# Issuing 18 on-chip moves from the sync engine, behind the fourth in-loop weight block, in a fused attention and mixture-of-experts kernel

## What is computed

```
for t in range(768):                     # decayed linear attention, 2 x 8 heads of 48
    y[t] = r[t] @ (state + (u * k[t]) v[t]^T)
    state = w * state + k[t] v[t]^T
x = y as 1536 tokens x 384 features
h = x @ w_in                             # 384 x 2048
x = (max(h, 0) + alpha * min(h, 0)) @ w_out
logits = x @ w_gate                      # 8 experts, the best one for each token, capacity 384
out[token] = gate * (relu(x @ w1[e]) @ w2[e])   # 384 x 1024 x 384 in each expert
```

## Time and profile before

| what | value |
|---|---|
| median of three runs | 447.54 us (447.43, 447.54, 448.78) |
| the profiled execution | 448.75 us |
| its span (first to last instruction) | 446.8 us |
| PE busy | 422.0 us, 94% |
| DVE, ACT, POOL busy | 257.8, 197.1, 176.3 us |
| mean granted TensorE clock | 0.984 of full speed |

### The profile page before, as it was taken

How to read it: one execution, slowest core, us unless ns; L and a number is a source line. 1 busy time by engine, 2 the same in 40 slices (tenths; PEclk the granted TensorE clock), 3 DMA queues, 4 the chain that set the end, 5 groups by cost and what they waited for, 6 DMA issues and landing times.

```text
span 446.8 us, 9384 instructions
## 1 busy us (share of the span) xinstructions
PE 422.0 (94%) x3333; PEld 408.4 (91%) x3333; DVE 257.8 (58%) x555; ACT 197.1 (44%) x450; POOL 176.3 (39%) x189
## 2 busy tenths in 40 slices
PE   5799999999999999999999986899999999998893
PEld 4688889999999999999999985699999999998893
DVE  6898867674445433633437663444568584648820
ACT  2789933432311122111323332344568684558731
POOL 4999625554324432244535861520110311011112
PEclk9999999999999999999999998899999999999998
DMA  7995035437950000000012440494686866564000
GB/s 249 404 353 185 3 112 162 135 94 266 371 199 19 35 1 0 0 35 18 0 35 84 140 148 17 160 352 135 193 229 195 259 197 198 159 213 109 10 19 7
DMA packets 33935, 61.45 MB, mean 138 GB/s; under 512 B 4654, under 2 KB 26910, under 8 KB 33888
## 3 DMA queue, kind: packets, MB, share of 16 engines
q1 hardware_dynamic: 31008, 55.53, 38.6%
q0 software_dynamic: 2880, 5.29, 3.5%
HBM read 47.53 MB, written 14.79 MB: 139 GB/s over the span
## 4 chain that ended last, share of the span: by engine, by line
PE 79%; DVE 7%; ACT 5%; issue 4%; POOL 2%; DMA 0%; POOLq 0%; ACTq 0%; DVEq 0%
PE bank L1154 20%; PE bank L1169 20%; PE bank L1279 18%; PE bank L1308 13%; ACT scores L613 3%; PE bank L1055 2%; PE bank L1266 1%; PE bank L1121 1%; ACT w_high L596 1%; DVE scores L828 1%; DVE neg L886 1%; PE bank L1085 1%; DVE act_full L892 1%; POOL k_hat L484 1%; PE bank L1113 1%
## 5 line engine op out<-in xcount | busy, mean ns | idle before, releaser
L512 POOL TENSOR_TENSOR g_low<-act_full,g_high 128x384 fp32r<-128x384 f32 x63 | 63.6, 1010 | 114.6 <-ACT g_high L642 114.6
L642 ACT ACTIVATE g_high<-act_full 128x384 fp32r<-128x384 f32 x64 | 33.7, 526 | 150.0 <-DVE act_full L892 137.3
L1154 PE MATMUL bank<-x_split,w_high 128*128 (+1 forms) x384 | 98.4, 337 | 0.0
L886 DVE TENSOR_SCALAR neg<-bank,alpha_sb 128x384 f32<-128x384 f32 x64 | 39.2, 613 | 71.5 <-PE bank L1154 71.4
L568 POOL DMA_INDIRECT out<-y_out,token x24 | 25.1, 1047 | 123.8 <-ACT y_out L729 120.1
L1154 PEld LDWEIGHTS bank<-x_split,w_high 128*128 128x128 f32 x384 | 69.0, 188 | 0.2 <-issue 0.2
L1169 PE MATMUL bank<-w_high,g_high 128*128 128x384 f32 x189 | 65.1, 344 | 1.1 <-POOL g_low L512 1.1
L1154 PE MATMUL bank<-x_split,w_low 128*128 (+1 forms) x192 | 64.4, 336 | 0.0
L1169 PE MATMUL bank<-w_high,g_low 128*128 128x384 f32 x189 | 63.8, 337 | 0.0
L1169 PE MATMUL bank<-w_low,g_high 128*128 128x384 f32 x189 | 63.7, 337 | 0.0
L1279 PE MATMUL bank<-xe_high,w_high 128*128 128x256 f32 (+1 forms) x192 | 58.6, 305 | 1.9 <-DVE xe_low L1005 1.9
(11 more groups left out here) (127 smaller groups left out, 793.7 us busy)
## 6 DMA issues: line engine op xcount, KB each, us to landing
w_raw<-chunks SPq DMA_DIRECT2D x96, 192.0 KB, 3.1
w_raw<-chunks SPq DMA_DIRECT2D x32, 384.0 KB, 3.1
rk_in<-att_rk SPq DMA_DIRECT2D x12, 704.0 KB, 6.3
routed_rows<-fill SPq DMA_DIRECT2D x1, 5211.0 KB, 17.1
xe<-routed_rows SPq DMA_DIRECT2D x7, 579.0 KB
v_in<-att_v SPq DMA_DIRECT2D x12, 200.0 KB, 6.2
out<-fill SPq DMA_DIRECT2D x1, 2304.0 KB, 23.4
x_split<-x_split POOLq DMA_DIRECT2D x18, 48.0 KB, 2.6
```

The source lines that it names most:

```text
L512: pool.tensor_tensor(gl[:, f % 4, :], act_full[:, f % 2, :], gh[:, f % 4, :].bitcast(f32), ALU.subtract).then_inc(s_gl, 1)
L642: act.activation(gh[:, f % 4, :], act_full[:, f % 2, :], ACT.Copy).then_inc(s_gh, 1)
L886: dve.tensor_scalar(neg[:, f % 2, :], h, 0.0, alpha_sb[:, f:f + 1], ALU.min, ALU.mult)\
L1154: last = mm(bank[f % 4][:, 0:G], a[:, f, w], x[:, kc, bass.ds(g * G, G)], start=kc == 0 and i == 0, stop=kc == KC - 1 and i == 2)
```

## The change

SP issues the 18 moves in one run, after weight blocks 4 to 7 and ahead of block 8. SP's first loop round is written out (its blocks are constants now), and the loop begins at block 8. POOL issues none of them, and its wait for `s_xl` goes with them. `move_piece`, the order of the 18 and their semaphore stay.

```diff
@@ sync engine
-            with sp.Fori(1, NF // RAW) as k:
+            for m in range(RAW):
+                load_chunk(RAW + m, m)
+
+            sp.wait_ge(s_xl, T)
+            for n in range((NG - 1) * 2 * KC):
+                move_piece(sp, 1 + n // (2 * KC), n % (2 * KC))
+            with sp.Fori(2, NF // RAW) as k:
                 for m in range(RAW):
                     load_chunk(RAW * k + m, m)
@@ gpsimd
             for f in range(NF):
                 g_low(0, f)
-                if f == 0:
-
-                    pool.wait_ge(s_xl, T)
-                for n in range(3 * f // 2, min(3 * (f + 1) // 2, (NG - 1) * 2 * KC)):
-                    move_piece(pool, 1 + n // (2 * KC), n % (2 * KC))
```

## The result

The changed kernel takes 455.34 us in the median of 4 runs (454.74 to 455.78), the kernel before 448.16 in runs beside it (447.43 to 448.79): ratio 1.0162, 95% interval 1.0143 to 1.0181, 7.2 us slower. Forecast were 454.5 (452.0 to 457.2) and +7.0. Its profiled execution has a span of 453.1 against 446.8, 6.3 longer. The four runs of the kernel before fall into two pairs, at 447.4 to 447.5 and at 448.8, and 448.16 is the middle between them. In the 19 to 25 runs of it beside each batch of experiments its median is 447.6 to 447.7; against that the change costs 7.6 to 7.7.

The account below looks back on a forecast made before the run. PE, busy 94% of the span, was taken to bound the kernel. Stall 5.6 plus clock 1.6 minus 0.2 given back made +7.0 us on the median 447.54, so 454.5, range 452.0 to 457.2.

Parts of the forecast that it names:

- What bounds the kernel, and the chain: First group: PE bounds; late block 8 delays ACT, DVE and POOL in turn, then the `down` of step 5, one stall.
- The run of issues: SP between blocks 7 and 8: 18 moves at 0.64 take 11.5 us; block 8 goes out at 78.1, 8.8 late.
- The landing: Block 8 lands 3.1 us after its issue (3.0 to 4.3), at 81.2; ACT wants it at 75.46.
- The stall: PE ahead of the `down` of step 5: it starts at 85.6 instead of 79.96, a stall of 5.6 us.
- The clock: PE's clock halves once after the stall, costing 1.6 us; bounds 0 and 2.8.
- rival (a): Block 8 late, but PE's clock stays up: +5.4 us, 452.9; chance 0.15.
- What is given back: First group after the stall: PE goes at 3.15 against the side loop's 3.19 a step, for -0.2 us.
- POOL's relief: POOL loses 18 issues, 9.5 us in all; worth 0 on the path, at most 0.4 to 0.5 us.
- (b): SP's issues as dear as its first move, 1.02 each with gap: 18.4 us in all, time 461.4; chance 0.08.
- (c): SP's issues cheap, 0.37 a move: block 8 only 0.9 late, 448.3, no measurable change; chance 0.07.
- (d): Block 8 in time, needing 0.32 a move; POOL's relief gains 0.4 to 0.5 us, 447.0; chance 0.04.
- The fills: Two table fills on SP go out at about 97.8 behind block 15 instead of 102.61; cost 0.

Follow-up runs that it names:

- e6: The changed kernel, but with SP's loop written out and block 9 issued only when block 8 has landed: 454.79 us, ratio 1.0152 to the kernel before.
- e8: The changed kernel, but with all 18 moves in one run on SP behind block 15 instead of block 7: 446.89 us, ratio 0.9981 to before.
- e3: The changed kernel, but with 12 moves behind block 7 and the other 6 behind block 15: 449.53 us, ratio 1.0029 to before.
- e2: The changed kernel, but with the same bytes at the same place in 6 wide transfers instead of 18: 450.08 us, ratio 1.0039 to before.
- e5: The kernel before, moves still on POOL, with 18 tiny loads added on SP between blocks 7 and 8: 451.36 us, ratio 1.0082.
- e4: The changed kernel with 44 extra transposes on PE in the stall ahead of the `down` of step 5: 457.29 us, ratio 1.0243 to before.
- e7: The kernel before without the 18 moves anywhere, so groups 1 to 3 have incomplete features: 446.17 us, ratio 0.9973.
- e9: The changed kernel, but with 9 moves on POOL and the other 9 in a run behind block 7 on SP: 447.96 us, ratio 1.0005 to before.
- e10: The changed kernel, but with one move on POOL and 17 spread over SP behind blocks 7 to 15: 446.4 us, ratio 0.9963 to before.
- e1: The changed kernel, but with the 18 moves on SP spread, two behind each of blocks 7 to 15: 446.8 us, ratio 0.9982 to before.

## Why the prediction came out right

**What bounds the kernel, and the chain.** Right, step by step: block 8, ACT's `w_high`, DVE's `w_low`, `neg` and `act_full`, `g_high`, `g_low`, the `down` of step 5. It was one stall, and no later block was late.

**The run of issues.** Forecast 18 x 0.64 = 11.5, SP free at 78.0; measured 11.80, free at 78.26. A single issue took 0.59; one gap of 0.4 in the middle of the run makes most of the difference. The way into the loop was taken for 0.1, for which no row stood, and took 0.50; written out (e6) it is 0.1. Block 8 went out at 78.76 against 78.1.

**The landing.** The term that was mis-sized most: 3.1 forecast, 4.05 measured, inside the bound of 4.3, but that bound came from other rows. It isn't the later blocks (e6). The excess sits in the issue of block 8, 1.18 instead of 0.33; it was long in all three kernels with 18 real moves ahead (0.96 to 1.42), and not with 12, 9 or 18 tiny loads. Block 5's issue and a move inside e8's run were as long, so the count ahead doesn't explain it alone. What SP waits for inside such an issue the trace doesn't name; that stays open.

**The stall.** ACT started on block 8 at 82.83 against 81.2: 0.26 for the run, 0.4 for the loop, 0.95 for the landing. The chain from there to PE was 0.16 shorter than forecast (4.24 against 4.4), so the `down` of step 5 started at 87.07 against 85.6. PE had run dry at 80.20, hence 6.87 idle and not 5.6.

**The clock.** Forecast one fall and 1.6 us; it came, and cost 2.2: from the `down` of step 5 to that of step 6 it is 5.35 (87.07 to 92.42) instead of 3.17 (79.96 to 83.13). The matmuls had the 0.32 spacing that the row of before gave; more of them were slow. The doubt in rival (a) was sound: around 2.30 and 2.56 us of idle time the clock fell (e3, e2), around 2.95 it stayed up (e5), each in one execution. And in the change and e6, where PE stood idle from the same 80.2 on, it fell at about 84.9 and about 82.7. So idle time alone doesn't tell.

**What is given back.** Forecast 0.2, measured 0.26 (from the `down` of step 6 to group 1 33.09 instead of 33.35). But it hangs on the clock: while PE was slow the side loop got ahead, and PE then went at its own 3.15. Where the clock stayed up, PE stayed at the loop's pace, and nothing was given back (e4: 33.36 for the same stretch).

**POOL's relief, taken as 0.** In the group this is right (e7). For the whole it was wrong by 1.5 us: I looked only at what stands behind POOL's issues in the group, not at the closing drain, which pays 0.081 us for each transfer that POOL issued (e9, e10). The trace of before showed the drain's 5.68 us, but not what it consists of.

**The sum.** The forecast's 5.65 + 1.6 - 0.2 stands against 7.11 + 2.2 - 0.3 = 9.0 in the group, then -1.5 for the drain: 7.5, which fits the 7.6 to 7.7 against the larger sample of before. In the two profiled executions another -1.4 comes from a fall of the clock at the experts that one had and the other hadn't. A stall taken 1.5 and a clock term taken 0.6 too small stood against a gain of 1.5 that I hadn't seen. That the total came so near is luck; that it is one stall, by this chain, and one fall of the clock is not.

**The rivals.** (a), a clock that stays up, didn't come in the profiled execution of the change, but did in e5 and e9. (b), 0.98 an issue, is refuted: the first of the 18 took 0.59 like the rest. (c) and (d) would have needed 0.37 and 0.32 an issue; even a load of 256 bytes cost 0.49. As the Trainium skill's page "DMA: Bandwidth & Descriptors", section "Issuing engines are not separate DMA queues", says, the transfers run on the same DMA engines whoever issues them, and only the issuing sequencer's time differs. e1 and e8 agree, moved issues are free there. The half sentence "usually small" is the one that a reader must check: 11.8 us for 18 issues here, ahead of a block with 3 to spare.

**The fills** went out early and held up nothing, as forecast.

## What to carry to other kernels

When transfers are moved to another engine's queue, multiply their number by that engine's price for one issue, and compare the product with the slack of the first thing behind them: the same 18 issues cost 9 us in the group at one place, and next to nothing when spread in pairs or put 26 us later. If there is a choice, put moves with no due time where the queue idles, and look at who stands behind whoever waits: the stall reached PE over three in-order engines. Compare landmarks over the whole trace, not only at the place of the edit; here the program's close moved with the edit, and the clock at the experts differed from one execution to the next.

## What the runs showed of the hardware that I had not expected

- POOL's drain at the end of the program grows by 0.08 us for each of these moves that POOL issued: 4.22, 4.30, 4.95 and 5.68 us with 0, 1, 9 and 18 moves.
- Six copies of 144 KB between SBUF partitions kept the DMA engines at a share of about 1.0 at 107 to 124 GB/s (e2, 70 to 76), and ACT got the block behind them 6.6 us after its issue; eighteen of 48 KB with the same bytes, at the issue rate of SP, left the engines at a share of 0.3 to 0.4 (the change, 72 to 78).
- SP's price of one issue depends on the transfer: 0.33 us for a block of 128 partitions, 0.42 in the median for a load of 256 bytes, 0.59 for a move of 16 partitions.
- Behind 18 moves the next issue took 0.96 to 1.42 us instead of 0.33; behind 12 it took 0.35. Single issues of over 1 us stand elsewhere too (a move inside e8's run 1.65, block 5 in the change 1.41).
- The clock fell around an idle time of 2.30 us (e3, just after PE had started again) and not around one of 2.95 us (e5). With PE idle from 80.2 on in both, it fell at about 84.9 in the change and at about 82.7 in e6.
